# Attention and two MLPs on one core: the first tile's square moved from VectorE to ScalarE in 25 of 192 periods

## The reference

```python
# attention over channels: q, k, v are (2, 6080, 256), tau a scalar
qn = q / (norm(q, axis=1) + 1e-6); kn = k / (norm(k, axis=1) + 1e-6)
a = softmax(kn^T @ qn / tau, axis=-1)          # 256 x 256 for each of the 2 batches
x = (v @ a).reshape(12160, 256)
# two MLPs, d_model 256, d_ff 2048
for w_in, w_out in (layer 1, layer 2):
    h = maximum(x @ w_in, 0)
    x = (h * h) @ w_out
```

## Time and profile before

| | us |
|---|---|
| runs shown, median (lowest to highest) | 2101.57 (2101.32 to 2105.85), 3 runs |
| the profiled execution's own time | 2102.23 |
| its span | 2100.4 |

### The profile page before, as it was taken

The page is one execution under the profiler, slowest core; times in us unless marked ns, Lnnn a source line. Parts: engine busy times, 40 slices in busy tenths (PEclk is TensorE's granted clock), DMA queues, the critical chain, the costliest instruction groups (busy, mean ns, idle before and its releaser), DMA issues.

```text
span 2100.4 us, 26208 instructions
## 1 busy us (share of the span) xinstructions
PE 2066.2 (98%) x9292; PEld 1723.8 (82%) x9292; DVE 1613.1 (77%) x2453; ACT 1202.4 (57%) x2071; POOL 2.7 (0%) x9
## 2 busy tenths in 40 slices
PE   8799999999999999999999999999999999999997
PEld 7688888888888888888888788888888888888886
DVE  6798888878778787777778877777777777777775
ACT  4566666666566555555556655555555555555553
POOL 0000000000000000000000000000000000000000
PEclk9899999999999999999999999999999999999999
DMA  8302022130201101011102011011011010110111
GB/s 273 85 11 71 31 81 60 41 90 23 62 25 41 31 11 41 20 20 30 47 5 89 21 41 41 1 41 39 1 41 37 4 41 24 17 41 1 40 20 20
DMA packets 233939, 86.90 MB, mean 41 GB/s; under 512 B 203440, under 2 KB 221872, under 8 KB 231248
## 3 DMA queue, kind: packets, MB, share of 16 engines
q1 hardware_dynamic: 233808, 85.23, 15.9%
HBM read 60.29 MB, written 24.90 MB: 41 GB/s over the span
## 4 chain that ended last, share of the span: by engine, by line
PE 94%; DVE 4%; ACT 1%; issue 1%; DMA 1%; SPq 0%; DVEq 0%; ACTq 0%
PE bank L360 16%; PE bank L359 16%; PE bank L361 16%; PE bank L350 14%; PE bank L351 14%; PE bank L352 14%; PE bank L510 2%; PE bank L476 1%; DVE gl L760 1%; DVE g_sb L787 1%; PE bank L442 1%; PE bank L440 1%; PE bank L438 1%; DMA qk<-in_k 0%; DVE wsl L760 0%
## 5 line engine op out<-in xcount | busy, mean ns | idle before, releaser
L359 PE MATMUL bank<-gh,oh 128*128 128x512 f32 (+1 forms) x1536 | 595.1, 387 | 1.3 <-DVE gl L760 0.7
L360 PE MATMUL bank<-gl,oh 128*128 128x512 f32 (+1 forms) x1536 | 594.9, 387 | 0.0
L361 PE MATMUL bank<-gh,ol 128*128 128x512 f32 (+1 forms) x1536 | 594.9, 387 | 0.0
L350 PE MATMUL bank<-xh,wsh 128*128 128x512 f32 (+1 forms) x1344 | 526.1, 391 | 11.5 <-DVE xl L760 7.2
L351 PE MATMUL bank<-xl,wsh 128*128 128x512 f32 (+1 forms) x1344 | 521.4, 388 | 0.0
L352 PE MATMUL bank<-xh,wsl 128*128 128x512 f32 (+1 forms) x1344 | 521.2, 388 | 0.0
L760 DVE TENSOR_TENSOR gl<-g_sb,gh 128x512 fp32r<-128x512 f32 (+1 forms) x768 | 491.9, 679 | 2.6 <-ACT gh L546 2.6
L546 ACT ACTIVATE gh<-g_sb 128x512 fp32r<-128x512 f32 (+1 forms) x768 | 460.2, 621 | 6.9 <-DVE g_sb L787 6.8
L546 ACT ACTIVATE p_sb<-bank 128x512 f32<-128x512 f32 (+1 forms) x384 | 227.8, 593 | 344.1 <-PE bank L352 343.9
L787 DVE SCALAR_TENSOR_TENSOR g_sb<-g_sb 128x512 f32<-128x512 f32 (+1 forms) x576 | 395.5, 687 | 19.7
L359 PEld LDWEIGHTS bank<-gh,oh 128*128 128x128 f32 x1536 | 288.3, 188 | 60.5 <-issue 1.9
(11 more groups left out here) (84 smaller groups left out, 955.5 us busy)
## 6 DMA issues: line engine op xcount, KB each, us to landing
v_sb<-in_v SPq DMA_DIRECT2D x160, 64.0 KB, 2.4
y_mid<-xf SPq DMA_DIRECT2D x10, 1024.0 KB, 4.8
xf<-y_mid SPq DMA_DIRECT2D x10, 1024.0 KB, 5.4
out<-xf SPq DMA_DIRECT2D x160, 64.0 KB, 2.2
raw<-in_q SPq DMA_DIRECT2D x22, 256.0 KB, 2.8
raw<-in_k SPq DMA_DIRECT2D x22, 256.0 KB, 3.4
qk<-in_q SPq DMA_DIRECT2D x10, 512.0 KB, 4.6
qk<-in_k SPq DMA_DIRECT2D x10, 512.0 KB, 5.6
```

Source lines behind the costliest of these rows:

```text
L350: nc.tensor.matmul(ps[:, 0:n], wsh[:, c, cols], ah, start=first, stop=False, skip_group_check=not first)
L359: nc.tensor.matmul(ps, oh[:, half, c, cols], gh[:, g, 0:n], start=first, stop=False)
L360: nc.tensor.matmul(ps, oh[:, half, c, cols], gl[:, g, 0:n], start=False, stop=False)
L361: return nc.tensor.matmul(ps, ol[:, half, c, cols], gh[:, g, 0:n], start=False, stop=last)
```

## The change

In the 25 periods for which `weights_made(k)` holds (0 to 7, 47 to 54, 95 to 103) C11 is no longer squared by VectorE. ScalarE does a Relu on the tile in place and then a Square in place, after `copy_u` and ahead of high11. A new semaphore orders the two. In the other 167 periods nothing changes.

```diff
+        c11_relu = sem("c11_relu")
...
+        def weights_made(k):
+            return w_chunk(k) is not None or o_chunk(k) is not None
...
+            def square11(Q):
+
+                n = width(Q // QUADS)
+                act.wait_ge(c11_added, Q + 1)
+                h = g_sb[:, F11, 0:n]
+                nc.scalar.activation(h, h, ACT.Relu).then_inc(c11_relu, 1)
+                act.wait_ge(c11_relu, sum(weights_made(q) for q in range(Q + 1)))
+                nc.scalar.activation(h, h, ACT.Square).then_inc(c11_sq, 1)
...
                 if up:
                     copy_u(k)
+                    if weights_made(k):
+                        square11(k)
                     high(k, G11, F11, c11_sq, d11_done, g11_hi)
...
                 if up:
                     add11(k)
-                    square(k, F11, c11_added, c11_sq)
+                    if not weights_made(k):
+                        square(k, F11, c11_added, c11_sq)
```

## The result

| | before | after |
|---|---|---|
| median of runs, us | 2103.10 (6 runs, 2101.32 to 2105.85) | 2110.64 (6 runs, 2109.64 to 2113.53) |
| ratio, 95% interval | | 1.0036 (1.0026 to 1.0046) |
| profiled execution, own time / span | 2102.23 / 2100.4 | 2109.64 / 2107.7 |

The change makes the kernel slower, by 7.5 us in the medians and 7.3 in the spans. The forecast was slower, 2106.5 within 2103.0 to 2110.0; the measured median lies 0.6 above the range. The profiled execution is the fastest of its six, so that what follows explains its 7.3 us.

The account below looks back on a forecast made before the run. TensorE's matmuls bound the kernel, with waits where wsl comes later than p1 needs it. First stage 3.4, second 3.0, restarts 0.6, third stage -2.1: +4.9 us, forecast 2106.5 us for the median, range 2103.0 to 2110.0.

Parts of the forecast that it names:

- the restart: On TensorE, each new stall also costs its first matmul about 0.07 us; nine stalls, +0.6 us.
- The rival with 1.04 for the pair: Relu and Square overlap on ScalarE, taking 1.04 instead of 1.32 us; kernel about 2104 us, chance 0.22 (or larger slack).
- Period 3: Fold period: low11 1.25 us later, add22 at 112.22 instead of 111.26, next p1 0.34 us later.
- period 0 +0.97: First period, already bound by the chain through add22 and wsl: copy_v moves by the full 0.97 us.
- 51 +1.22: Unit 6: later transposes delay the weight transfer, fold +0.92 us; then transposes again, +0.30.
- third stage -2.1: Periods 95 to 102, without a fold: the freed 0.73 us of vector queue counts; 2.1 us gained in all.
- The freed vector time: 0.73 us per period on VectorE; does nothing in period 3, where the weight combination waits for take_fold.
- Period 1: 0: Fold period with nothing between low11 and add22: add22 0.5 us later, wsl still before p1, no cost.
- The second stage as a sum of waits: Periods 47 to 54: waits in 50 to 54 add 3.02 us, before the extra 0.07 for each new stall.
- Slack taken as zero cost: Periods 47, 48, 49: copy_v sets add22 0.5 us later, wsl still arrives 0 to 0.2 before p1; cost 0.
- The rule: Where wsl bounds the period, the next p1 is never earlier than add22's start + 2.57 us.
- The first rival: Each scalar hand-over costs 0.09 us, not 0.04: +7 to +8.5 us, about 2109 us; chance 0.20.

Follow-up runs that it names:

- vector_refilled: The changed kernel with a vector instruction of the old square's form and size put back on a scratch tile in the 25 periods; single run 2111.23 us.

## Why the prediction was right or wrong

Right, step by step:

- *The place and sign.* The loss is in the fold periods, through high11, low11, add22, wsl and p1, and the gain in 95 to 102; no stretch outside moved but the start of the first period and period 55, which pays the restart of its own p1.
- *The pair's price*: 0.66 for each, measured 0.66 to 0.67, as the next instruction starts 0.03 after the end of the one it needs. The rival with 1.04 for the pair falls. The Trainium skill (ScalarE: Activation LUTs, "What ACT_TABLE_LOAD costs") has back-to-back ACTIVATEs overlap by about 93 ns; the trace shows that for independent ones (wsh starts 0.09 ahead of high11's end in period 3), not across this dependency.
- *Period 3*: low11 was forecast 1.25 later and came 7.99 after p1 instead of 6.63, 1.36 later; 0.07 to 0.1 of that is the restart that the sum had as a term of its own.
- *Terms*: period 0 +0.97 forecast (+1.01 at its wait), 2 +0.33 (+0.42), 3 +0.34 (+0.41), 4 +0.96 (+1.04), 5 +0.60 (+0.77), 6 +0.21 (+0.25), 50 +0.33 (+0.35), 51 +1.22 (+1.29), 52 +0.43 (+0.58), 53 +0.81 (+0.95 to +0.98), 54 +0.23 (+0.35), third stage -2.1 (-1.96). Most of the small excess is the restart's 0.07, which was one lump of 0.6 in the sum; so are the 0.10 and 0.12 of periods 7 and 55.
- *The freed vector time is worthless beside a fold*: shown by vector_refilled.

Wrong:

- *Period 1: 0.* This is the step that failed: the sum costs a longer wait of TensorE at the wait's own length and puts nothing on what comes behind it. Period 0's wait of 1.20 became 2.20, as forecast, and the clock fell behind it; period 1 grew by 0.87, with a pair of its own or without, and not at all where period 0 had no such wait. The profile of before had the lower level at p1 of period 0, where matmuls follow a wait of 7.20, and I did not ask what a longer wait elsewhere would do.
- *The second stage as a sum of waits, +3.3 with the restarts.* The profile gave +3.8; in two of four profiles the fall of the clock at period 51's fold adds 1.4 to 1.6 more. (Of its 1.27 us of waiting before, names 1.11; 1.27 is the distance to the fold less a plain one.) The forecast saw the transfer coming later, priced it as 0.92 of waiting, and stopped there. No rival held such a fall, so the range had no room for it.
- *Slack taken as zero cost.* Periods 47, 48 and 49 grew by 0.05, 0.10 and 0.10: add22 in 48 came at 9.30 and 9.30 + 2.57 is the 11.87 measured. The rule was right; add22 moved by 0.66 (from 8.64 after p1), not by 0.5, and the slack did not cover it.
- *The base.* The forecast stood on 2101.57, the median of three runs; six gave 2103.10. That is 1.5 of the 4.1 us between forecast and result; the other 2.6 would have stood inside the range. The median is 0.64 outside, so without either of the two, this 1.5 or period 1's 0.87, it would have been inside.
- *The first rival's number.* The 7.5 us lie in its +7 to +8.5, but not for its reason: the pair's hand-overs measured 0.03 to 0.04, not 0.09.

The likeliest reading of the 7.3 us between the spans: 4.9 as forecast, 1.3 more in the first stage (0.87 of it in period 1, shown to come from the pair in period 0, and 0.21 in period 0 ahead of the wait, where the clock rose later), about 0.6 of small terms in the second and in period 55, 0.1 less gain in the third, 0.3 in the start, which other profiles show to scatter by more: 7.2. What stays open is how often the clock falls in period 51 in timed runs of the whole change, and why equal waits end at different levels.

## What to carry to other kernels

In a queue that is worked off in order the place of an instruction can count more than its length: 1.3 us of scalar work in each of 25 periods cost 7.5 us behind copy_u and nothing a few instructions earlier, where the engine was waiting for another. Before moving work off a busy engine, look for who waits next on the engine that takes it, and put it into that engine's longest wait whose inputs are ready. And when a change lengthens a wait of TensorE, price the matmuls after it at the lower clock as a case of its own.

## What the runs showed of the hardware

- A wait of TensorE of 2.20 us in period 0 was followed by matmuls 0.42 to 0.43 us apart instead of 0.227; the period behind it took 12.84 to 13.10 in the four kernels with the pair in period 0 behind copy_u (12.92, 12.89, 12.84, 13.10), and 12.03 to 12.06 in the eight others, whose wait there was 1.19 to 1.54.
- At period 51 waits of 2.02 and 2.07 us ended at the full level and waits of 1.99 and 2.05 us at the lower, in four kernels whose code in these periods differs in nothing that TensorE or ScalarE does.
- Dependent scalar instructions of 0.63 us start 0.66 to 0.67 apart; independent ones 0.54 (high11 112.66 to wsh 113.20, in period 3 of after).
